# Low parts, token loads and the fifth group's norm in another order in a channel mixer on one core

## The chip, the cores and the metric

The kernel runs on one core of a Trainium2 chip. The metric is device time in microseconds (us) of the whole program. The engines are PE (TensorE, matrix products), DVE (VectorE), ACT (ScalarE), POOL (GpSimd) and SP (SyncE, which here only issues DMA transfers).

## The reference

Three stages follow each other. The first is a linear attention with softmaxes over q and k; its output is x. The second and third are the ones that the change touches:

```python
def _moe_ref(x, w_tok1, w_tok2, w_ch1, w_ch2):
    h = np.maximum(x.transpose(0, 2, 1) @ w_tok1, 0.0) @ w_tok2
    u = x + h.transpose(0, 2, 1)
    h2 = np.maximum(u @ w_ch1, 0.0) @ w_ch2          # 512 -> 1536 -> 512   ("stage B")
    return u + h2

def _moe2_ref(x, g_ln, w_ch1, w_ch2):
    mu = np.mean(x, axis=-1, keepdims=True)
    var = np.mean((x - mu) ** 2, axis=-1, keepdims=True)
    xn = (x - mu) / np.sqrt(var + 1e-06) * g_ln
    ch = np.maximum(xn @ w_ch1, 0.0) @ w_ch2         # 512 -> 2048 -> 512   ("stage C")
    return x + ch
```

There are 8 x 576 = 4608 tokens of 512 channels, all in fp32.

## The kernel before

**Phase A** (up to about 224 us of the span) does the attention and the token mixing. **The plain stage** (224 to 350 us) does stage B for the first of five token groups with ordinary products, in 12 units of weights, while the weights of stages B and C are prepared for the rest.

**The calls** (350 us to the end) do the other nine positions: position 1 to 4 is stage B for token groups 1 to 4, position 5 to 9 is stage C for all five groups. A group is 2 x 462 tokens (2 x 456 for the last). A large product of 2 x 2 blocks is done with seven block products instead of eight (Winograd's form), so that each call has seven products p = 0 to 6. A position has a few *mixing-in calls* j = 0, 1, ... (three in B, four in C; the product with w1) and then one *w2 call* (j < 0; the product with w2). Each product of a mixing-in call is one *entry*; each product of a w2 call is three entries in B and four in C. One entry is one weight tile of 512 KB in a ring of four (`w_ring`) and twelve matmuls. Entries of a call are counted from 0 (n).

Every operand stands as a high part and a low part (`x_hi` and `x_lo`, `o_hi` and `o_lo`): three matmuls (lines 1445 to 1447) make one exact product of them. ACT writes the high part, and DVE then the low one as the difference. The operands of x are seven (p = 0 to 6); four sums (`sum_x`) on DVE stand between them. Each of the nine positions prepares the x of the next one: p = 0 to 3 in the last mixing-in call, the rest behind it. The operands of the hidden layer are made entry by entry (`hi_o` on ACT, `lo_o` on DVE, line 1308), with `sum_o` (lines 1294 to 1302) before products 2, 4 and 6. `take` (ACT line 886, DVE line 1278) brings a product from PSUM to the hidden layer, `relu` (line 892) and `relu_t1` (line 1285) finish it, and `take_y` (line 1320) adds the products of a w2 call to the result. PE may start product p when product p - 2 has been taken.

All order is written out by hand. Each engine runs through the calls in the same order of steps, and executes its own instructions strictly one after another; semaphores tie them. SP issues, at each entry, first the weight tile four entries on (when PE is done with this entry), then what else falls there: `load_x` (line 428; the four quarters of the x of two positions on, into the single tile `xn`), `load_res` (line 473), and stores of y. All of these go through SP's one DMA queue. POOL adds the weight blocks and stores and loads the weight units (lines 590, 557, 558) through its own queue.

**The norm** of stage C is spread over the mixing-in calls of the position before, by the table `NORM_AT`: (j, p) is the call and product at which each step stands. Its mean and variance are sums over channels made by PE (`moment 0`, `moment 1`, four small matmuls each). The first row of the table is for the norm of position 5, which is made during position 4 (here "the fifth's norm"); the other row is for the later ones. `HI_AT` is the list of entries at which ACT makes the high parts of a weight unit; its last number is that of the last unit, in position 4.

Of the kernel before, what the change touches and what calls it, by code (L numbers as in the profile page):

```python
# [8 lines left out]
def mixer_kernel(nc, q, k, kT, v, w_tok1, w_tok2, w1b, w2b, g_ln, w1c, w2c, out):  # L9
# [45 lines left out]
    for pos in range(1, NX):  # L55
        stage, sg = "BC"[pos // NSG], pos % NSG
        for j in range(G1S[stage] + 1):
# [19 lines left out]
         "deviation 0": (0, 4), "deviation 1": (0, 4), "deviation 2": (0, 5), "deviation 3": (0, 5),  # L77
         "square 0": (0, 5), "square 1": (0, 5), "square 2": (0, 5), "square 3": (0, 5),
         "squares 01": (0, 6), "squares 23": (0, 6), "squares": (0, 6), "second high": (0, 6), "second low": (1, 0),
         "moment 1": (1, 2), "variance": (1, 3), "root": (1, 3), "newton": (1, 4),  # L80
         "scaled 0": (1, 5), "scaled 1": (1, 5), "scaled 2": (1, 6), "scaled 3": (1, 6)},
# [6 lines left out]
    HI_AT = ((0, 8, 27), (1, 6, 11, 27), (1, 6, 11, 27), (4,))  # L88
# [72 lines left out]
    with ctx:  # L161
# [201 lines left out]
        def _(sp):  # L363
# [159 lines left out]
            for c in CALLS:  # L523
                for n in range(7 * c.epp):
# [9 lines left out]
                    if c.j == 0 and c.pos == 1 and p in (2, 3, 4, 5):  # L534
                        load_x(2, p - 2)
                    if c.j < 0 and c.pos + 2 < NX and c.pos != NSG - 1 and p in (2, 3, 4, 5) and e == 0:
                        load_x(c.pos + 2, p - 2)
# [139 lines left out]
        def _(act):  # L677
# [70 lines left out]
            def plain(n):  # L748
# [25 lines left out]
                for p in {7: (0, 1), 8: (2, 3), 9: (4, 5), 10: (6,)}.get(n, ()):  # L774
                    hi_x(1, p)
# [156 lines left out]
            for c in CALLS:  # L932
# [21 lines left out]
                else:  # L954
                    for n in range(7 * c.epp):
# [4 lines left out]
                        if c.pos + 1 < NX and n in (c.epp, c.epp + 2):  # L960
                            hi_x(c.pos + 1, 5 + (n > c.epp))
# [3 lines left out]
        def _(dve):  # L965
# [165 lines left out]
            def plain(n):  # L1131
# [17 lines left out]
                if n == 6:  # L1149
                    sum_x(1, 0)  # L1150
                    lo_side(2)
                if n == 7:
                    lo_x(1, 0)
                    lo_x(1, 1)
                    sum_x(1, 1)
                if n == 8:
# [3 lines left out]
                if n == 9:  # L1160
# [3 lines left out]
                if n == 10:  # L1164
# [220 lines left out]
            for c in CALLS:  # L1385
                after = CALLS[c.index + 1] if c.index + 1 < len(CALLS) else None
                split = c.pos + 1 < NX
                if c.j >= 0:
                    last = c.j == G1S[c.stage] - 1
                    for p in range(7):  # L1390
                        if p == 0 and c.j > 0:
                            relu_t1(CALLS[c.index - 1])
                        if p in (3, 4, 5):
# [12 lines left out]
                        if last and split and p == 4:  # L1406
                            lo_x(c.pos + 1, 2)
                            lo_x(c.pos + 1, 3)
                        if last and p == 5:
                            lo_o(after, 0, 0)  # L1410
                            lo_o(after, 0, 1)
                        if last and split and p == 6:
                            lo_x(c.pos + 1, 4)
                        if last and p == 6 and after.epp > 3:
                            lo_o(after, 0, 2)
                else:
                    for n in range(7 * c.epp):
# [12 lines left out]
                        if split and n == c.epp:  # L1430
                            lo_x(c.pos + 1, 5)
# [285 lines left out]
```

## Time and profile before

| | us |
|---|---|
| median of 3 runs | 1524.27 (1522.53 to 1527.17) |
| the profiled execution, its own time | 1519.46 |
| span of the profiled execution (first to last instruction) | 1517.7 |
| PE busy | 1475.5 (97%) |
| DVE busy | 1048.5 (69%) |
| ACT busy | 687.0 (45%) |
| POOL busy | 266.9 (18%) |

The profiled execution is 4.8 us below the median of the runs. A PE matmul is shown with a modelled duration that overlaps the next one, so its pace is read from start to start and not from the duration.

### The profile page before, as it was taken

The page shows a single profiled execution, that of the slowest core. Times are in us where ns is not written, and L with a number is a line of the kernel's source. Part 1 is how long each engine was busy: PE and PEld are TensorE (multiplying, and loading weights), DVE is VectorE, ACT ScalarE, POOL GpSimd, SP SyncE. Part 2 cuts the span into 40 slices and gives each one's busy share as a digit, 9 for nine tenths or more (in the row PEclk, how much of TensorE's full clock was granted, in tenths as well). Part 3 has the DMA queues.
Part 4 walks back from the last instruction along what each step waited for, and adds up shares of the span by engine and source line. Part 5 has one row for each costly group of instructions (what it writes and reads, how often), then busy time and mean ns, then how long its engine had stood idle before and what let it go on. Part 6 is the DMA issues. An engine that isn't in the chain of part 4 may idle for free.

```text
span 1517.7 us, 19961 instructions
## 1 busy us (share of the span) xinstructions
PE 1475.5 (97%) x7656; PEld 1331.4 (88%) x7656; DVE 1048.5 (69%) x1187; ACT 687.0 (45%) x862; POOL 266.9 (18%) x280
## 2 busy tenths in 40 slices
PE   6999999998999999999999999999999999999998
PEld 6999998887888888888888888888888888889997
DVE  7989874593693782785975786588568756872276
ACT  5656564452543633634533443454245324532342
POOL 5454656652121222110000000000000000000000
PEclk9999999999999999999999999999999999999999
DMA  7788849889889999987777768766866787678766
GB/s 240 244 265 243 277 167 332 334 319 368 310 326 313 371 328 312 342 320 256 251 261 265 239 227 271 238 233 236 277 238 219 257 257 254 203 232 249 250 210 201
DMA packets 138719, 407.27 MB, mean 268 GB/s; under 512 B 13568, under 2 KB 35392, under 8 KB 138624
## 3 DMA queue, kind: packets, MB, share of 16 engines
q1 hardware_dynamic: 123024, 347.00, 68.1%
q0 software_dynamic: 15600, 58.99, 10.5%
q8 instruction: 62, 1.02, 0.3%
q14 instruction: 33, 0.27, 0.1%
HBM read 326.24 MB, written 79.69 MB: 267 GB/s over the span
## 4 chain that ended last, share of the span: by engine, by line
PE 81%; DMA 8%; DVE 6%; issue 2%; POOL 1%; ACT 1%; SPq 0%; DVEq 0%; ACTq 0%; POOLq 0%
PE ps L1445 26%; PE ps L1447 26%; PE ps L1446 25%; DMA w_ring<-w_scratch_B 4%; DMA w_scratch_B<-w_out 3%; PE ps L1469 1%; DVE x_lo L1066 1%; PE ps L1560 1%; PE ps L1480 1%; DVE o_lo L1308 1%; DMA vt<-v 0%; DVE k_max L971 0%; DVE w_out L1113 0%; DVE kv L1027 0%; DVE h L1278 0%
## 5 line engine op out<-in xcount | busy, mean ns | idle before, releaser
L1445 PE MATMUL ps<-x_hi,w_ring 128*128 128x462 f32 (+1 forms) x920 | 343.9, 374 | 12.6 <-DMA w_ring<-w_scratch_B 7.8
L1445 PE MATMUL ps<-o_hi,w_ring 128*128 128x462 f32 (+1 forms) x920 | 343.1, 373 | 5.8 <-DVE o_lo L1308 3.2
L1447 PE MATMUL ps<-x_hi,w_ring 128*128 128x462 f32 (+1 forms) x920 | 342.8, 373 | 0.0
L1446 PE MATMUL ps<-o_lo,w_ring 128*128 128x462 f32 (+1 forms) x920 | 341.6, 371 | 0.0
L1447 PE MATMUL ps<-o_hi,w_ring 128*128 128x462 f32 (+1 forms) x920 | 341.5, 371 | 0.0
L1446 PE MATMUL ps<-x_lo,w_ring 128*128 128x462 f32 (+1 forms) x896 | 333.5, 372 | 0.0
L907 ACT CAST o_hi<-h 128x924 fp32r<-128x924 f32 (+1 forms) x189 | 182.0, 963 | 235.3 <-PE ps L1447 223.5
L1308 DVE TENSOR_TENSOR o_lo<-h,o_hi 128x924 fp32r<-128x924 f32 (+1 forms) x189 | 212.4, 1125 | 63.2 <-ACT o_hi L907 63.1
L1445 PEld LDWEIGHTS ps<-x_hi,w_ring 128*128 128x128 f32 x920 | 173.5, 189 | 38.2 <-issue 13.0
L1445 PEld LDWEIGHTS ps<-o_hi,w_ring 128*128 128x128 f32 x920 | 173.1, 188 | 32.8 <-issue 12.3
L1447 PEld LDWEIGHTS ps<-x_hi,w_ring 128*128 128x128 f32 x920 | 173.4, 188 | 19.5
L1446 PEld LDWEIGHTS ps<-o_lo,w_ring 128*128 128x128 f32 x920 | 173.2, 188 | 19.2
L1447 PEld LDWEIGHTS ps<-o_hi,w_ring 128*128 128x128 f32 x920 | 173.0, 188 | 19.2
L1278 DVE TENSOR_TENSOR h<-ps,h 128x924 f32<-128x924 f32 (+1 forms) x81 | 90.5, 1117 | 139.0 <-PE ps L1447 138.8
L1446 PEld LDWEIGHTS ps<-x_lo,w_ring 128*128 128x128 f32 x896 | 169.5, 189 | 19.0
L886 ACT ACTIVATE h<-ps 128x924 f32<-128x924 f32 (+1 forms) x108 | 101.4, 940 | 179.6 <-PE ps L1447 179.5
L892 ACT ACTIVATE h<-h 128x924 f32<-128x924 f32 (+1 forms) x54 | 52.7, 975 | 161.7 <-DVE h L1278 161.7
L1320 DVE TENSOR_TENSOR res<-ps,res 128x924 f32<-128x924 f32 (+1 forms) x63 | 70.1, 1113 | 55.0 <-PE ps L1447 54.3
L1066 DVE TENSOR_TENSOR x_lo<-xn,x_hi 128x924 fp32r<-128x924 f32 (+1 forms) x63 | 70.9, 1139 | 22.0 <-ACT x_hi L798 22.0
L798 ACT CAST x_hi<-xn 128x924 fp32r<-128x924 f32 (+1 forms) x63 | 59.3, 957 | 11.0 <-DVE xn L1050 7.1
L590 POOL DMA_DIRECT2D w_scratch_C<-w_out x13 | 12.5, 960 | 282.2 <-DVE w_out L1171 282.2
L907 ACT CAST o_hi<-last_pair 128x924 fp32r<-128x924 f32 (+1 forms) x35 | 33.8, 965 | 45.3 <-PE ps L1447 45.3
(172 smaller groups left out, 2132.7 us busy)
## 6 DMA issues: line engine op xcount, KB each, us to landing
w_ring<-w_scratch_C SPq DMA_DIRECT2D x280, 512.0 KB, 3.8
w_ring<-w_scratch_B SPq DMA_DIRECT2D x168, 512.0 KB, 5.0
w_scratch_C<-w_out POOLq DMA_DIRECT2D x13, 1792.0 KB, 11.4
w_scratch_B<-w_out POOLq DMA_DIRECT2D x12, 1792.0 KB, 10.6
kt<-kT SPq DMA_DIRECT2D x32, 288.0 KB, 6.1
u_scratch<-u_out SPq DMA_DIRECT2D x32, 288.0 KB, 3.3
qt<-q SPq DMA_DIRECT2D x32, 256.0 KB, 4.8
ke<-k SPq DMA_DIRECT2D x32, 256.0 KB, 5.0
```

The source lines that it names most:

```text
L798: nc.scalar.copy(x_hi[:, p, :, 0:n], x).then_inc(x_hi_made, 1)
L886: nc.scalar.activation(hidden(dst, c.j, c.n), bank[:, :, 0:c.n], func)\
L892: nc.scalar.activation(x, x, ACT.Relu).then_inc(relu_made, 1)
L907: nc.scalar.copy(o_hi[:, g % RO, :, 0:c.n], hidden((0, 1, 1, 2, 0, 3, 3)[p], e, c.n)).then_inc(o_hi_made, 1)
L1066: nc.vector.tensor_tensor(x_lo[:, p, :, 0:n], x, x_hi[:, p, :, 0:n], ALU.subtract)\
L1278: nc.vector.tensor_tensor(x, bank[:, :, 0:c.n], x, ALU.add).then_inc(taken["dve"], 1)
L1308: nc.vector.tensor_tensor(o_lo[:, g % RO, :, 0:c.n], src, o_hi[:, g % RO, :, 0:c.n], ALU.subtract)\
L1320: nc.vector.tensor_tensor(y, bank[:, :, 0:c.n], y, ALU.add).then_inc(taken["dve"], 1)
L1445: mm(dst, a_hi, b_hi, start=start, stop=False, skip_group_check=onto)
L1446: mm(dst, a_hi, b_lo, start=False, stop=False, skip_group_check=onto)
L1447: return mm(dst, a_lo, b_hi, start=False, stop=stop, skip_group_check=onto)
L1469: x = mm(dst, ke[:, t, c * P:(c + 1) * P], vt[:, t, c // 2, c % 2 * P:c % 2 * P + P + 1], start=t == 0, stop=t == NT - 1)
```

## The change

It changes no computation, only when things are done, in five places.

1. DVE, last mixing-in call of each position: the low part of the w2 call's first operand (`lo_o(after, 0, 0)`) stands before the take of product 5 and not behind it; `lo_x` 3, 4, 5, `sum_x` 3 and `lo_x` 6 each move back, to product 6 and to entries epp, epp + 1, epp + 2 and epp + 4 of the w2 call (epp is 3 in B and 4 in C). ACT makes the high part 6 one entry later.
2. SP, w2 calls: the four quarters of the x of two positions on are loaded at products 3, 4, 5, 6 and not at 2, 3, 4, 5.
3. SP, position 1: the four quarters for position 2 are loaded at entries 4, 6, 8, 10 and not at 2, 3, 4, 5.
4. The fifth's norm: deviations and squares one product earlier, "second high" behind the take of product 0 of call j = 1, variance, root, newton and the scalings one product earlier; the last weight unit's high part at entry 0 and not 4.
5. Plain stage: x operands one unit later.

```diff
-         "deviation 0": (0, 4), "deviation 1": (0, 4), "deviation 2": (0, 5), "deviation 3": (0, 5),
-         "square 0": (0, 5), "square 1": (0, 5), "square 2": (0, 5), "square 3": (0, 5),
-         "squares 01": (0, 6), "squares 23": (0, 6), "squares": (0, 6), "second high": (0, 6), "second low": (1, 0),
-         "moment 1": (1, 2), "variance": (1, 3), "root": (1, 3), "newton": (1, 4),
-         "scaled 0": (1, 5), "scaled 1": (1, 5), "scaled 2": (1, 6), "scaled 3": (1, 6)},
+         "deviation 0": (0, 3), "deviation 1": (0, 3), "deviation 2": (0, 4), "deviation 3": (0, 4),
+         "square 0": (0, 3), "square 1": (0, 3), "square 2": (0, 4), "square 3": (0, 4),
+         "squares 01": (0, 5), "squares 23": (0, 5), "squares": (0, 6), "second high": (1, 0), "second low": (1, 0),
+         "moment 1": (1, 2), "variance": (1, 2), "root": (1, 2), "newton": (1, 3),
+         "scaled 0": (1, 4), "scaled 1": (1, 4), "scaled 2": (1, 5), "scaled 3": (1, 5)},
...
-    HI_AT = ((0, 8, 27), (1, 6, 11, 27), (1, 6, 11, 27), (4,))
+    HI_AT = ((0, 8, 27), (1, 6, 11, 27), (1, 6, 11, 27), (0,))
...
-                    if c.j == 0 and c.pos == 1 and p in (2, 3, 4, 5):
-                        load_x(2, p - 2)
-                    if c.j < 0 and c.pos + 2 < NX and c.pos != NSG - 1 and p in (2, 3, 4, 5) and e == 0:
-                        load_x(c.pos + 2, p - 2)
+                    if c.pos == 1 and (c.j, p) in ((0, 4), (0, 6), (1, 1), (1, 3)):
+                        load_x(2, ((0, 4), (0, 6), (1, 1), (1, 3)).index((c.j, p)))
+                    if c.j < 0 and c.pos + 2 < NX and c.pos != NSG - 1 and p in (3, 4, 5, 6) and e == 0:
+                        load_x(c.pos + 2, p - 3)
...
+                        if last and p == 5:
+                            lo_o(after, 0, 0)
+                        if last and p == 6 and after.epp > 3:
+                            lo_o(after, 0, 2)
                         if p in (3, 4, 5):
                             take(c, p)
...
                         if last and split and p == 4:
                             lo_x(c.pos + 1, 2)
-                            lo_x(c.pos + 1, 3)
                         if last and p == 5:
-                            lo_o(after, 0, 0)
                             lo_o(after, 0, 1)
                         if last and split and p == 6:
-                            lo_x(c.pos + 1, 4)
-                        if last and p == 6 and after.epp > 3:
-                            lo_o(after, 0, 2)
+                            lo_x(c.pos + 1, 3)
...
                         if split and n == c.epp:
+                            lo_x(c.pos + 1, 4)
+                        if split and n == c.epp + 1:
                             lo_x(c.pos + 1, 5)
-                        if split and n == c.epp + 1:
+                        if split and n == c.epp + 2:
                             sum_x(c.pos + 1, 3)
-                        if split and n == c.epp + 2:
+                        if split and n == c.epp + 4:
                             lo_x(c.pos + 1, 6)
```

The first place is SP's list at the start of the calls, position 1. `w_ring` is a weight tile, `y_scratch<-res` a store of the plain stage's result, `xn` a quarter of the x of position 2. Before:

```order
L463 DMA w_ring<-w_scratch_B 128x1024
L485 DMA y_scratch<-res 128x924 x4
L463 DMA w_ring<-w_scratch_B 128x1024 x3
L428 DMA xn<-u_scratch 128x924
L463 DMA w_ring<-w_scratch_B 128x1024
L428 DMA xn<-u_scratch 128x924
L463 DMA w_ring<-w_scratch_B 128x1024
```

In the change:

```order
L463 DMA w_ring<-w_scratch_B 128x1024 x5
L428 DMA xn<-u_scratch 128x924
L463 DMA w_ring<-w_scratch_B 128x1024 x2
L428 DMA xn<-u_scratch 128x924
L463 DMA w_ring<-w_scratch_B 128x1024 x2
```

The tiles of entries 7 and 8 had one and two quarters of x ahead of them that are now behind them.

The second place is DVE's list at the end of a last mixing-in call in stage C (takes of products 4 and 5 are the `last_pair` rows of L1278). Before:

```order
L1278 TENSOR_TENSOR last_pair<-ps,last_pair 128x924
L1066 TENSOR_TENSOR x_lo<-xn,x_hi 128x924 x2
L1278 TENSOR_TENSOR last_pair<-ps,last_pair 128x924
L1308 TENSOR_TENSOR o_lo<-h,o_hi 128x924 x2
L1066 TENSOR_TENSOR x_lo<-xn,x_hi 128x924
```

In the change (its lines stand one or two further down):

```order
L1279 TENSOR_TENSOR last_pair<-ps,last_pair 128x924
L1066 TENSOR_TENSOR x_lo<-xn,x_hi 128x924
L1309 TENSOR_TENSOR o_lo<-h,o_hi 128x924
L1279 TENSOR_TENSOR last_pair<-ps,last_pair 128x924
L1309 TENSOR_TENSOR o_lo<-h,o_hi 128x924 x2
L1066 TENSOR_TENSOR x_lo<-xn,x_hi 128x924
```

The first `o_lo` of the w2 call has changed places with the fourth `x_lo`; the take of product 5 still has two instructions ahead of it, and the second `o_lo` still follows that take.

The third place is ACT's list in the fifth's norm, from the takes of products 0 and 1 of call j = 0 in position 4 on. L782 is the last weight unit's high part, L892 a relu, L919 the squares, L923 "second high". Before:

```order
L886 ACTIVATE h<-ps 128x2x456 x2
L916 CAST s_hi<-ln 128x924
L886 ACTIVATE h<-ps 128x2x456
L892 ACTIVATE h<-h 128x2x456
L782 CAST w_out<-w_op 128x7x256
L892 ACTIVATE h<-h 128x2x456
L919 ACTIVATE ln<-xn 128x924 x4
L886 ACTIVATE h<-ps 128x2x456
L923 CAST s_hi<-ln 128x924
L886 ACTIVATE h<-ps 128x2x456 x3
```

In the change:

```order
L782 CAST w_out<-w_op 128x7x256
L886 ACTIVATE h<-ps 128x2x456
L916 CAST s_hi<-ln 128x924
L886 ACTIVATE h<-ps 128x2x456
L919 ACTIVATE ln<-xn 128x924 x2
L892 ACTIVATE h<-h 128x2x456
L919 ACTIVATE ln<-xn 128x924 x2
L892 ACTIVATE h<-h 128x2x456
L886 ACTIVATE h<-ps 128x2x456 x2
L923 CAST s_hi<-ln 128x924
L886 ACTIVATE h<-ps 128x2x456 x2
```

The take of product 0 of call j = 1 (the second of the last "x2" before "second high") now stands ahead of "second high", and the squares are split in two pairs.

## Rows read from the trace of the kernel before

**Rows 1.** The page: busy time by engine; the chain that ended last.

```profile
PE 1475.5 (97%) x7656; PEld 1331.4 (88%) x7656; DVE 1048.5 (69%) x1187; ACT 687.0 (45%) x862; POOL 266.9 (18%) x280
...
PE 81%; DMA 8%; DVE 6%; issue 2%; POOL 1%; ACT 1%; SPq 0%; DVEq 0%; ACTq 0%; POOLq 0%
```

**Rows 2.** Windows: length, busy (count) by engine, granted clock, DMA share, GB/s.

```profile
362.00:370.00 8.00, 6.83 (x33) 5.80 (x32) 3.36 (x3) 2.89 (x3) 0.70 (x1) 1.00 1.03 420
713.79:718.00 4.21, 4.21 (x13) 3.72 (x14) 0.27 (x1) 0.77 (x1) 0.00 (x0) 0.59 0.86 311
900.00:1000.00 100.00, 100.00 (x478) 89.48 (x477) 65.08 (x61) 37.48 (x40) 0.00 (x0) 1.00 0.78 258
```

**Rows 3.** SP and PE timeline, position 1: start, length, engine, instruction.

```profile
357.92 0.42 SPq L428 DMA_DIRECT2D xn<-u_scratch  x1
360.05 0.32 SPq L463 DMA_DIRECT2D w_ring<-w_scratch_B  x1
360.42 0.81 SPq L428 DMA_DIRECT2D xn<-u_scratch  x1
...
369.88 0.45 PE L1445 MATMUL ps<-x_hi,w_ring 128*128 128x462 f32 x1 [1.17 <-DMA w_ring<-w_scratch_B]
...
372.27 0.37 PE L1447 MATMUL ps<-x_hi,w_ring 128*128 128x462 f32 x1
374.40 0.44 PE L1445 MATMUL ps<-x_hi,w_ring 128*128 128x462 f32 x1 [1.76 <-DMA w_ring<-w_scratch_B]
```

**Rows 4.** The chain in order of time around 370 us.

```profile
363.73 10.54 DMA w_ring<-w_scratch_B
```

**Rows 5.** Timeline around the start of the w2 call of position 5.

```profile
868.60 2.14 DVE L1066 TENSOR_TENSOR x_lo<-xn,x_hi 128x924 fp32r<-128x924 f32 x2
870.66 1.11 DVE L1278 TENSOR_TENSOR last_pair<-ps,last_pair 128x924 f32<-128x924 f32 x1
871.69 1.11 DVE L1308 TENSOR_TENSOR o_lo<-h,o_hi 128x924 fp32r<-128x924 f32 x1
872.21 0.38 PE L1447 MATMUL ps<-x_hi,w_ring 128*128 128x462 f32 x1
872.95 0.45 PE L1445 MATMUL ps<-o_hi,w_ring 128*128 128x462 f32 x1 [0.36 <-DVE o_lo L1308]
...
873.66 1.12 DVE L1308 TENSOR_TENSOR o_lo<-h,o_hi 128x924 fp32r<-128x924 f32 x1 [0.87 <-ACT o_hi L907]
```

**Rows 6.** Windows of DVE: second low part to that of entry 6, w2 calls, B.

```profile
409.56:424.08 14.52, 14.52 (x15) 1.00 0.79 272
519.49:534.66 15.17, 14.61 (x15) 1.00 0.82 284
```

**Rows 7.** DVE and PE timeline around entry 8, w2 call of position 1.

```profile
428.23 1.11 DVE L1308 TENSOR_TENSOR o_lo<-h,o_hi 128x924 fp32r<-128x924 f32 x1
...
429.49 0.45 PE L1445 MATMUL ps<-o_hi,w_ring 128*128 128x462 f32 x1
```

**Rows 8.** Windows of PE, entries 6 to 14 of the w2 calls of positions 1 and 3.

```profile
424.23:448.53 24.30, 23.39 (x109) 1.00 0.93 338
...
647.84:671.82 23.98, 23.20 (x108) 1.00 0.91 327
```

**Rows 9.** Timeline of DVE, ACT and PE in the fifth's norm.

```profile
710.79 1.12 DVE L1366 TENSOR_TENSOR ln<-ln 128x924 f32<-128x924 f32 x1
...
711.94 0.96 ACT L923 CAST s_hi<-ln 128x924 fp32r<-128x924 f32 x1 [2.03 <-DVE ln L1366]
712.81 1.75 ACT L886 ACTIVATE h<-ps 128x912 f32<-128x912 f32 x2
...
710.03 0.37 PE L1447 MATMUL ps<-x_hi,w_ring 128*128 128x456 f32 x1
713.79 0.47 PE L1445 MATMUL ps<-x_hi,w_ring 128*128 128x456 f32 x1 [3.39 <-ACT h L886]
```

**Rows 10.** DVE timeline, the first of the three steps of "newton", and the take before.

```profile
723.95 1.11 DVE L1278 TENSOR_TENSOR h<-ps,h 128x912 f32<-128x912 f32 x1 [0.35 <-PE ps L1447]
724.97 1.11 DVE L1375 TENSOR_TENSOR ln<-ln 128x924 f32<-128x924 f32 x1
```

More of the change, by code:

```diff
@@ L773, in plain @@
                     hi_side(2)
-                for p in {7: (0, 1), 8: (2, 3), 9: (4, 5), 10: (6,)}.get(n, ()):
+                for p in {8: (0, 1), 9: (2, 3), 10: (4, 5), 11: (6,)}.get(n, ()):
                     hi_x(1, p)
@@ L959, in _ @@
                             hi_unit(HI_AT[c.e0 + n])
-                        if c.pos + 1 < NX and n in (c.epp, c.epp + 2):
+                        if c.pos + 1 < NX and n in (c.epp, c.epp + 3):
                             hi_x(c.pos + 1, 5 + (n > c.epp))
@@ L1149, in plain @@
                 if n == 6:
-                    sum_x(1, 0)
                     lo_side(2)
                 if n == 7:
+                    sum_x(1, 0)
+                if n == 8:
                     lo_x(1, 0)
@@ L1155, in plain @@
                     sum_x(1, 1)
-                if n == 8:
+                if n == 9:
                     lo_x(1, 2)
@@ L1159, in plain @@
                     lo_x(1, 3)
-                if n == 9:
+                if n == 10:
                     lo_x(1, 4)
@@ L1163, in plain @@
                     sum_x(1, 3)
-                if n == 10:
+                if n == 11:
                     lo_x(1, 6)
```

## The prediction

> **What bounds the kernel now.** I read the page first: PE is busy for 97% of the span and holds 81% of the chain that ended last; DMA holds 8% and DVE 6% [rows 1]. So only what makes PE wait counts. The windows give PE's undisturbed pace: 478 matmuls in 100 us, 0.21 us each, 2.52 us for an entry of twelve [rows 2]. I then went through PE's starts and looked at each step longer than 0.21 us. Those steps are few, and the change touches four sets of them.
>
> (a) In position 1 entries 7 and 8 start at 369.88 and 374.40, each on a landed weight tile [rows 3]. The second start comes 2.13 us after the matmul before it and so is 1.92 late; the first is 1.34 late: its row shows 1.17 of idleness behind a modelled end that lies 0.16 (0.37 - 0.21) after the free start, as 1.76 + 0.16 gives the 1.92 of the second. The tile of entry 8 took 10.54 us to land [rows 4].
>
> (b) At the start of the w2 calls of positions 1 to 8 (eight times) PE's step is about 0.74 us, 872.21 to 872.95, and the row names the low part o_lo as releaser [rows 5]. That is 0.53 late. A first matmul after a wait also has a step of about 0.28 and not 0.21, so a wait costs 0.6 in all.
>
> (c) In the w2 calls of positions 1 to 3 the nine entries from entry 6 on take 24.30 us (position 1) and 23.98 (position 3), against 9 x 2.52 = 22.7 [rows 8]; position 2 is like them. Most of the 1.3 to 1.6 us excess is weight tiles that land late, at entry 12 above all, with DMA at 91% and 93% of its time.
>
> (d) In the fifth's norm PE steps from 710.03 to 713.79, 3.55 us late, and waits for a take on ACT [rows 9]. That take stood behind "second high", which waited 2.03 us for the sum of squares on DVE. Right behind the wait the granted clock is 0.59 on average over 4.21 us, in which 13 matmuls fit where 20 would (4.21 / 0.21) [rows 2]; part of that stretch is at 1.2 GHz, half the full 2.4.
>
> **The change, part by part.**
>
> *Weight tiles of position 1.* A quarter of x is 128 x 924 x 4 bytes, 0.47 MB; at the 420 GB/s of 362 to 370 us it takes 1.1 us, and about twice that while POOL's queue carries a weight store too [rows 2]. The quarters issued at 357.92 and 360.42 stand in SP's queue ahead of the tiles of entries 7 (issued 360.05) and 8 [rows 3]. With both behind, tile 7 comes up to 2.2 us sooner, more than the 1.34 that it is late, and tile 8 some 4 us sooner, more than the 1.34 + 1.92. The quarters now fall at entries 4, 6, 8 and 10, one every 5 us, and x is wanted only at entry 14, three entries (7.6 us) after the last. Gain 3.3 and 2 x 0.08 of slow first matmuls: **3.5**. If the tiles are late for POOL's store and not for x, it is 0; the whole is 3.5.
>
> *Start of the w2 calls.* DVE runs two x_lo (868.60, 2.14 us), the take (870.66), then o_lo (871.69), whose end at 872.80 releases PE 0.15 us later [rows 5]. In the change o_lo stands after the first x_lo and ends at about 870.7, 1.7 us before PE's free start at 872.42. The take stays where it was, behind two instructions. What is late next is the second low part: it waits for ACT (relu of product 5, then the high part), as before at 873.66, ends at 874.78 and lets PE go at 874.93, where PE wants 872.42 + 2.52 = 874.94 [rows 5]. It just fits. In C DVE then has gaps, and the wait vanishes in four calls: 4 x 0.6 = **2.3**. Bounds 0 and 2.4.
>
> In B it does not pay. From the second low part to that of entry 6 DVE works 14.52 of 14.52 us in position 1 [rows 6]; positions 3 and 4 are the same within 0.13. The change puts the same number of instructions into this stretch, which begins when the second high part is there, at the old time. So PE starts the w2 call 0.5 sooner and waits it off by entry 6. Only position 2 has a gap there, 15.17 - 14.61 = 0.56 [rows 6], a take_y that waited for a load; SP issues that load after entry 1, now 0.5 sooner: **0.5**.
>
> *The seventh x_lo in B.* It leaves entry 5 (sum_x 3 takes the place) for entry 7, where it stands behind a weight unit's low part and ahead of take_y and the low part of entry 8. That one ends at 429.34 now and PE starts on it at 429.49 [rows 7], already 0.15 late. One DVE instruction more, 1.03 from start to start as between 870.66 and 871.69 [rows 5], makes PE 1.03 later in positions 1, 2 and 3. If nothing else changed this would cost **3.1**.
>
> *x loads a product later.* In the same calls the first quarter stood ahead of the tile of entry 12, the late one. Behind it, that tile lands at least 1.1 sooner, and PE comes 1.03 later to it. The excess of the nine entries (1.6, 1.4 and 1.3) should shrink to the DVE wait alone, 0.15 + 1.03 + 0.08 = 1.26: gains of 0.4, 0.15 and 0.05, **0.6** after the 3.1 is paid. Later, at entry 18, the queue carries only tiles and one store; x is next wanted in the following position (stage C: at its call 0, three entries on; the fifth's norm: two entries and a take_y on, some 6 us).
>
> *The fifth's norm.* The take of product 0 now precedes "second high", so PE's 3.55 wait goes, and with it the slow stretch: 4.21 - 13 x 0.21 = 1.5 [rows 2, 9]. The squares come one product earlier too. New: the three steps of newton now stand between the takes of products 3 and 4. By my count PE runs product 2 at 710.2, its moment ends at 713.7, variance 715.0, root 716.0, take 3 at 716.2 to 717.3, newton 717.2 to 720.65 (three at 1.15, like the one at 724.97 [rows 10]), take 4 ends 721.7, and PE wants it at 721.0: 0.9 late. Bounds 0 and 2.5 (all three steps plus the take, none hidden). Gain 5.05 - 0.95: **4.1**. The Trainium skill (TensorE: Matmul & The Clock Gate, section "Part 1: The HAM clock gate") says that the number of slow matmuls at the start of activity differs from run to run; by that the 1.5 need not be paid in every run, and the sum would be 9.5 in the runs that escape it. One trace can't tell.
>
> *Plain stage.* The x operands move by one unit of 10 us; the last low part ends some 3 us before PE's first call. Nothing: the cover is that unit's products. Without cover it would be 1 us.
>
> Sum: 3.5 + 2.3 + 0.5 + 0.6 + 4.1 = **11.0**. The profiled execution's 1519.46 becomes 1508.5; the median of the runs stands 4.8 above its profile, and the same 11.0 off it is **1513.3**. What this kernel's measurement can tell from no change is about 0.3%, 4.6 us.
>
> **The rivals.**
>
> *The queue keeps its debt.* DMA is at 91 to 103% in all these stretches [rows 2, 8]; tiles may be late because of the total. Then (a) gives nothing and the three entry-8 waits are paid in full on top of the late tiles: 11.0 - 3.5 - 3.7 = 3.8, time 1520.5, no telling from before. Against it: where PE runs without a wait DMA needs 78% of its time [rows 2], so what is moved out of a crowded stretch finds room in the next. Chance 0.10.
>
> *DVE hands the wait on.* The second low part has a margin of 0.01; if it comes 0.3 to 0.6 late in C, (b) is worth 0 to 1. With newton at its worst, 2.5, the sum is 11.0 - 2 - 1.5 = 7.5, time 1516.8. For it: DVE without a gap in B [rows 6]. Chance 0.18.
>
> *SP stands still: slower.* The first quarter of x waits on SP for the seventh x_lo, and the weight tiles queue behind it. Now x_lo 6 is at entry 7 and the quarter at entry 9, six calls of this kind. If x_lo 6 ended after the tiles' reserve (entry 9, plus three tiles in the ring), each us would be PE's. By rows 7 it ends near 428.3 and SP gets there near 434.8, so 6.5 us are spare, and the ring's reserve on top. It decides only from 2.6 us of PE time per call (6 x 2.6 = 15.6, over 11.0 + 4.6): time 1529. Chance 0.03.
>
> *It doesn't act.* Each of PE's waits has another cause just behind, and all but the norm's 4.1 stays: 1520.2. Chance 0.05.
>
> **How the numbers follow.** The forecast has 0.64. Its own range is 1510.5 to 1515.5 (the bounds of newton and of C). The range of 1509.5 to 1520 takes in the DVE rival and most of the queue's. Faster by over 0.3% means below 1519.7: 0.64 + 0.18 and a little of the others, 0.84; slower 0.04; same 0.12.
>
> **What would show it.** PE's step at 369.88 and 374.40 back to 0.21; the eight w2 calls of B and C starting without a wait, entry 6 in B as late as before; a new wait of about 1.2 at entry 8 in positions 1 to 3 and none at entry 12; no clock below 1.00 near 714; a wait of some 0.9 before product 6 of call j = 1 of position 4. I am wrong if entries 7 to 9 of position 1 still wait for DMA, or if PE's time at entry 12 in B is later than before.

## The result and the profile after

The changed kernel takes 1517.4 us (median of 11 runs, 1509.66 to 1519.65) against 1524.3 for the kernel before in the same comparison (11 runs, 1521.35 to 1533.88). The ratio is 0.995, 95% interval 0.9936 to 0.9964: faster by 7.6 us of 1524.27, with the interval from 5.5 to 9.8. The forecast was 11.0 us and 1513.3.

The profiled execution of the changed kernel took 1519.06, which is 1.7 above its median, while that of the kernel before was 4.8 below its own. So the two traces differ by 1.2 us of span (1517.7 and 1516.5) where the medians differ by 6.9. The traces can show single waits. They can't show the total.

The page of the changed kernel: span; busy time by engine; the chain; and the two groups of matmuls that begin an entry, where the last columns are idle time ahead of them and what ended it. For these two groups the rows of the kernel before stand ahead. Lines of the changed kernel stand one or three further down: 1448 to 1450 are the three matmuls, 1309 is `lo_o`, 1279 the take on DVE, 1321 `take_y`.

```profile
span 1516.5 us, 19961 instructions
...
PE 1473.3 (97%) x7656; PEld 1330.2 (88%) x7656; DVE 1047.1 (69%) x1187; ACT 686.8 (45%) x862; POOL 265.3 (17%) x280
...
PE 69%; DMA 5%; DVE 4%; issue 1%; ACT 0%; SPq 0%; DVEq 0%
...
L1445 PE MATMUL ps<-x_hi,w_ring 128*128 128x462 f32 (+1 forms) x920 | 343.9, 374 | 12.6 <-DMA w_ring<-w_scratch_B 7.8 <-ACT h L886 3.4 <-issue 1.4
L1445 PE MATMUL ps<-o_hi,w_ring 128*128 128x462 f32 (+1 forms) x920 | 343.1, 373 | 5.8 <-DVE o_lo L1308 3.2 <-issue 1.8 <-DMA w_ring<-w_scratch_B 0.5
...
L1448 PE MATMUL ps<-x_hi,w_ring 128*128 128x462 f32 (+1 forms) x920 | 343.6, 373 | 9.5 <-DMA w_ring<-w_scratch_B 7.9 <-issue 1.0 <-DVE h L1279 0.6
L1448 PE MATMUL ps<-o_hi,w_ring 128*128 128x462 f32 (+1 forms) x920 | 343.2, 373 | 8.6 <-DVE o_lo L1309 6.6 <-issue 1.0 <-DMA w_ring<-w_scratch_B 1.0
```

PE does the same matmuls as in [rows 1]. ACT's 3.4 us, the take of the fifth's norm, is gone. The waits for weight tiles are not less in total: 7.9 and 1.0 us, where the kernel before has 7.8 and 0.5. Those for low parts have grown from 3.2 to 6.6 us: the waits at the starts of the w2 calls are gone and others, inside the w2 calls of stage B, have come, as the next views show.

From PE start to PE start, the two traces compare so (us, before and after; "6 to 9" are the entries n of a w2 call):

| stretch | pos. 1 | pos. 2 | pos. 3 | pos. 4 |
|---|---|---|---|---|
| mixing-in calls | 59.13, 56.06 | 55.12, 55.81 | 58.48, 58.55 | 59.80, 55.75 |
| w2 call, entries 0 to 6 | 15.39, 15.92 | 16.04, 16.98 | 15.37, 17.00 | 15.26, 15.80 |
| 6 to 9 | 7.86, 8.89 | 7.85, 8.91 | 7.85, 8.90 | 7.55, 7.66 |
| 9 to 15 | 16.44, 16.52 | 16.21, 15.50 | 16.14, 15.35 | 14.91, 14.91 |
| 15 to the next position | 15.12, 15.12 | 15.12, 15.12 | 15.12, 15.12 | 15.55, 17.03 |

The first row runs to the start of the w2 call and so holds the wait there, 0.50 to 0.55 in the kernel before. The mixing-in calls of positions 5 to 8 are shorter by 0.59, 0.57, 0.51 and 0.50. Phase A is 1.06 longer and the plain stage 0.61 shorter. Over the fourteen traces these two vary by 3.5 and 3.2 us, though every edit lies behind phase A. The plain stage has one of the five edits; no kernel here makes that one alone. It takes 119.9 us on average in the five traces without the edit and 119.0 in the nine with it, single traces 117.5 to 120.7, so a gain of 1 us there is neither shown nor excluded. A single difference below about 1 us in this table is no evidence by itself; one that repeats in three or four places is.

Timeline of the changed kernel around the start of the w2 call of position 5, to hold against [rows 5]:

```profile
869.55 1.11 DVE L1066 TENSOR_TENSOR x_lo<-xn,x_hi 128x924 fp32r<-128x924 f32 x1
870.58 1.12 DVE L1309 TENSOR_TENSOR o_lo<-h,o_hi 128x924 fp32r<-128x924 f32 x1
871.61 1.12 DVE L1279 TENSOR_TENSOR last_pair<-ps,last_pair 128x924 f32<-128x924 f32 x1
...
872.73 0.38 PE L1448 MATMUL ps<-x_hi,w_ring 128*128 128x462 f32 x1
873.37 0.37 PE L1448 MATMUL ps<-o_hi,w_ring 128*128 128x462 f32 x1
```

The two PE rows are three matmuls apart, 0.64 = 3 x 0.21: the w2 call starts without a wait, its low part having ended 1.7 earlier, at 871.70. This is so in all eight.

Timeline of the changed kernel around entry 8 in position 1, to hold against [rows 7]:

```profile
423.96 1.21 DVE L1172 TENSOR_TENSOR w_out<-w_op,w_out 128x1024 fp32r<-128x1024 f32 x1
425.10 1.11 DVE L1066 TENSOR_TENSOR x_lo<-xn,x_hi 128x924 fp32r<-128x924 f32 x1
426.13 1.11 DVE L1321 TENSOR_TENSOR res<-ps,res 128x924 f32<-128x924 f32 x1
427.16 1.10 DVE L1309 TENSOR_TENSOR o_lo<-h,o_hi 128x924 fp32r<-128x924 f32 x1
...
428.41 0.45 PE L1448 MATMUL ps<-o_hi,w_ring 128*128 128x462 f32 x1 [1.02 <-DVE o_lo L1309]
```

DVE has no gap; the second row is the seventh x_lo. PE starts 1.17 late here (a step of 1.38 from start to start, less 0.21), 1.18 and 1.15 in positions 2 and 3.

SP, PE and the chain of the changed kernel, start of position 1, to hold against [rows 3, 4] (in the last row: start and duration of the transfer):

```profile
357.99 5.81 SPq L463 DMA_DIRECT2D w_ring<-w_scratch_B  x3
363.85 0.60 SPq L428 DMA_DIRECT2D xn<-u_scratch  x1
366.00 2.86 SPq L463 DMA_DIRECT2D w_ring<-w_scratch_B  x2
368.91 0.44 SPq L428 DMA_DIRECT2D xn<-u_scratch  x1
...
374.88 0.45 PE L1448 MATMUL ps<-x_hi,w_ring 128*128 128x462 f32 x1 [1.38 <-DMA w_ring<-w_scratch_B]
...
366.00 8.75 DMA w_ring<-w_scratch_B
```

Entries 7 and 8 start freely. The tile of entry 9 has one quarter of x ahead of it (three in the kernel before), took 8.75 us, and makes PE 1.54 late, since PE now comes to it sooner.

The fifth's norm in the changed kernel, to hold against [rows 9, 10]: timeline rows of DVE, ACT and PE.

```profile
709.67 1.12 DVE L1367 TENSOR_TENSOR ln<-ln 128x924 f32<-128x924 f32 x1
...
711.76 0.93 ACT L886 ACTIVATE h<-ps 128x912 f32<-128x912 f32 x1 [2.36 <-PE ps L1450]
712.59 0.95 ACT L923 CAST s_hi<-ln 128x924 fp32r<-128x924 f32 x1
...
708.99 0.44 PE L1448 MATMUL ps<-x_hi,w_ring 128*128 128x456 f32 x1 [0.63 <-DMA w_ring<-w_scratch_B]
...
723.39 1.12 DVE L1380 SCALAR_TENSOR_TENSOR ln<-ln 128x924 f32<-128x924 f32 x1
724.43 1.10 DVE L1279 TENSOR_TENSOR h<-ps,h 128x912 f32<-128x912 f32 x1
...
725.59 0.48 PE L1448 MATMUL ps<-x_hi,w_ring 128*128 128x456 f32 x1 [0.58 <-DVE h L1279]
```

ACT now takes first and waits only for PE, so the wait of 3.55 is gone. Two small ones are there instead: 0.78 for a weight tile at product 0 (708.99) and 0.74 for the take behind newton (725.59). Windows of the changed kernel (columns as in [rows 2]):

```profile
611.74:615.80 4.06, 4.06 (x12) 3.53 (x13) 3.46 (x4) 0.35 (x1) 0.96 (x1) 0.58 0.93 364
...
708.00:718.00 10.00, 9.37 (x46) 8.21 (x45) 5.33 (x6) 5.36 (x7) 0.00 (x0) 1.00 0.76 266
```

The clock stays at 1.00 through the norm. A stretch at 0.58 has appeared at 611.74, behind a wait of 1.98 for a weight tile that the trace of before does not have.

### The profile page after: what moved, and what is told of

Read it like the earlier page. It is cut to its first block, busy times and chain, and to the rows that moved or that the text cites. A ratio compares the mean times of both kernels' runs of the same rounds, so it can differ in the third digit from the quotient of the medians.

```text
span 1516.5 us, 19961 instructions
## 1 busy us (share of the span) xinstructions
PE 1473.3 (97%) x7656; PEld 1330.2 (88%) x7656; DVE 1047.1 (69%) x1187; ACT 686.8 (45%) x862; POOL 265.3 (17%) x280
## 4 chain that ended last, share of the span: by engine, by line
PE 69%; DMA 5%; DVE 4%; issue 1%; ACT 0%; SPq 0%; DVEq 0%
PE ps L1448 23%; PE ps L1450 23%; PE ps L1449 23%; DMA w_ring<-w_scratch_B 5%; DVE o_lo L1309 2%; DMA res<-u_scratch 1%; DVE x_lo L1066 1%; DVE h L1295 1%; DVE res L1321 0%; DVE h L1279 0%; PE ps L1597 0%; PE ps L1598 0%; DVE w_out L1172 0%; DVE h L1286 0%; ACT h L892 0%
## 5 line engine op out<-in xcount | busy, mean ns | idle before, releaser
L892 ACT ACTIVATE h<-h 128x924 f32<-128x924 f32 (+1 forms) x54 | 52.7, 975 | 158.1 <-DVE h L1279 158.0
```

The lines of the kernel that those rows point to most:

```text
L892: nc.scalar.activation(x, x, ACT.Relu).then_inc(relu_made, 1)
```

## The experiments

My theory of the gain was the four terms of the prediction. The rivals were that only some of them act, and that weight tiles in crowded stretches keep their lateness whatever is moved. The first four kernels do one part of the change each, on the kernel before; the plain stage's edit has no such kernel.

**DVE order alone** (edit 1 of the change, nothing else).

> The kernel before with the new DVE order alone (first o_lo ahead of the take, x_lo 3 to 6 and sum_x 3 moved back). Theory (each of PE's waits has its own cause and adds up): the eight waits at the start of a w2 call vanish; in stage C this gives 4 x 0.6 = 2.3 us and stays; in stage B it is waited off by entry 6, and entry 8 of positions 1 to 3 waits 1.2 us (3 x 1.03 more), part of which the late weight tiles behind it cover. Sum between 2.3 faster and 0.8 slower, about 1 us faster. Rival (DVE hands the wait on): the second product of the w2 calls in C waits 0.3 to 0.6 us instead, and the whole is 1 to 3 us slower.

Measured: 1523.11 (12 runs), ratio 1.0002 [0.9983, 1.0021]. In the trace the C calls start 0.56, 0.57, 0.54 and 0.50 sooner, and entry 8 is late by 1.18 and 1.16 in positions 2 and 3. In position 1 it is only 0.19 late: PE had waited 2.0 at entry 5 and then ran at a clock of 0.66 for 5 us, while DVE went on. So entry 8 costs 2.2 in this trace and 3.1 where it is late three times. Against the 2.2 won in C that leaves no gain, as measured.

**Position 1's x loads alone** (edit 3).

> The kernel before with the x loads of position 1 alone moved to entries 4, 6, 8 and 10. Theory: entries 7 and 8 start without a wait, 3.5 us faster, visible in the mixing-in calls of position 1 and nowhere else. Rival (the queue keeps its debt): the same tiles or the next ones are late by as much, total within 1 us of before. The changed kernel's trace already shows entry 9 waiting 1.54 us, so I expect 2 to 3 us rather than 3.5.

Measured: 1521.29 (12 runs), 0.9974 [0.9959, 0.9988]: faster by 4.0, interval 1.8 to 6.2. The trace gives 2.2 of it in position 1 (59.13 to 56.91): the tiles of entries 7 and 8 land 7.2 and 7.3 us after their issue, not 9.7 and 10.5. It also shows where the rest of the forecast 3.5 stayed, in one PE row of its timeline, entry 9:

```profile
375.88 0.45 PE L1445 MATMUL ps<-x_hi,w_ring 128*128 128x462 f32 x1 [1.48 <-DMA w_ring<-w_scratch_B]
```

**x loads of the w2 calls alone** (edit 2).

> The kernel before with the x loads of the w2 calls alone at products 3 to 6. Theory: the late tile at entry 12 of positions 1 and 3 comes in time, 1.3 + 1.1 + 1.1 us less at most over positions 1 to 3; about 2 us faster. Rival (the queue keeps its debt): tiles are late elsewhere, no change. Second rival: the later x loads meet the weight store of the next position's first unit and cost there, 0 to 2 us slower.

Measured: 1522.16 (12 runs), 0.9985 [0.9969, 1.0001]: no gain shown. The first quarter of x now stands behind the tile of entry 12, which lands in 7.6 us in position 1, not 8.3. But in this trace the tile of entry 14 is then the late one (PE timeline, position 1):

```profile
447.70 0.47 PE L1445 MATMUL ps<-o_hi,w_ring 128*128 128x462 f32 x1 [1.11 <-DMA w_ring<-w_scratch_B]
```

Position 1 waits 0.38 and 1.26 at the two, position 2 0.31 and 1.19. Over three positions in each of the traces, entries 9 to 15 take 16.26 us on average with the old loads (four kernels), and 16.22 and 16.57 with the new ones (four kernels, and this one). So the lateness as a whole did not shrink. That the order moved it from one tile to the next is not shown: in position 1 the tile of entry 12 takes 8.1 us on average in the four traces with the old loads and 8.2 in the ten with the new, and entry 14 is late in some traces with the old loads too (1.09 in the kernel with the norm alone).

**The fifth's norm alone** (edit 4).

> The kernel before with the fifth's norm (and the last weight unit) alone moved. Theory: the 3.55 us wait and the slow clock behind it go, a wait of 0.75 before product 6 of call j = 1 comes, 4 us faster in the mixing-in calls of position 4. Rival (the last weight unit's store, now 14 us earlier, makes weight tiles late): a further wait of about 0.8 us at product 0 of call j = 1, as the changed kernel's trace has it, 3.3 us faster.

Measured: 1521.07 (12 runs), 0.9977 [0.9961, 0.9993]: faster by 3.5, interval 1.1 to 5.9. Position 4's mixing-in calls go from 59.80 to 56.60. Waits of 1.07 at product 0 and 0.73 behind newton, as in the changed kernel. The other three kernels of this group keep the old norm. In each the wait of 3.55 stands there again with a slow clock behind it; windows of the kernels with the DVE order alone and with position 1's x loads alone:

```profile
724.85:729.06 4.21, 4.21 (x13) 3.70 (x14) 0.27 (x1) 0.77 (x1) 0.00 (x0) 0.59 0.86 296
...
716.08:720.29 4.21, 4.21 (x11) 3.73 (x12) 0.27 (x1) 0.77 (x1) 0.00 (x0) 0.50 0.87 310
```

The next four kernels take one suspected fault out of the changed kernel each.

**The seventh x_lo at entry 9 in stage B.**

```diff
-                        if split and n == c.epp + 4:
+                        if split and n == c.epp + (4 if c.epp > 3 else 6):
                             lo_x(c.pos + 1, 6)
```

> The changed kernel with x_lo 6 in stage B two entries later still (entry 9, where no weight unit's low part stands ahead of it; stage C as it is). Theory: the wait of 1.17 us before entry 8 of positions 1, 2 and 3 comes from this one DVE instruction and falls to 0.15; products 6 to 8 of these w2 calls take 7.86 and not 8.9 us. The late weight tiles at entries 12 and 14 may take up to 1 us each of it back: 1 to 3 us faster than the changed kernel, 0.6 to 0.7% under the kernel before. Rival (the wait is DVE's whole backlog): it moves to entry 9 or 10 and nothing is won.

Measured: 1510.97 (6 runs), 0.9925 [0.99, 0.995]. Its timeline at the place shown above:

```profile
426.21 1.11 DVE L1321 TENSOR_TENSOR res<-ps,res 128x924 f32<-128x924 f32 x1
427.24 1.11 DVE L1309 TENSOR_TENSOR o_lo<-h,o_hi 128x924 fp32r<-128x924 f32 x1
...
428.15 0.37 PE L1450 MATMUL ps<-o_hi,w_ring 128*128 128x462 f32 x1
428.50 0.45 PE L1448 MATMUL ps<-o_hi,w_ring 128*128 128x462 f32 x1
```

PE's step is 0.35: 0.14 late, as in [rows 7], and not 1.17. Entries 6 to 9 take 7.85 us in all three positions, 1.04, 1.06 and 1.05 less than in the changed kernel. Nothing behind it takes the 3.1 back: entries 9 to 15 average 16.20 in the traces without this wait and 16.22 in those with it. By the ratio the gain over before is 11.4 (7.6 to 15.2) against 7.6 (5.5 to 9.8). The two intervals overlap, so it is the trace that shows the 3.1, and the times agree with it.

**The `res` load out of entry 1.** In the changed kernel DVE's take_y at entry 5 of positions 2 and 3 waits for a quarter of `res` that SP loads after entry 1. Timeline of the changed kernel, position 2:

```profile
527.14 1.11 DVE L1295 TENSOR_TENSOR h<-h 128x924 f32<-128x924 f32 x1
530.05 1.12 DVE L1321 TENSOR_TENSOR res<-ps,res 128x924 f32<-128x924 f32 x1 [1.80 <-DMA res<-u_scratch]
...
532.35 0.45 PE L1448 MATMUL ps<-o_hi,w_ring 128*128 128x462 f32 x1 [1.12 <-DVE o_lo L1309]
```

```diff
-                    if c.stage == "B" and c.j == 2 and p in (2, 4, 6):
-                        load_res(c.pos, p // 2 - 1)
-                    if c.stage == "B" and c.j < 0 and n == 1:
-                        load_res(c.pos, 3)
+                    if c.stage == "B" and c.j == 2 and p in (0, 2, 4, 6):
+                        load_res(c.pos, p // 2)
```

> The changed kernel with the last quarter of the result tile in stage B loaded with the others, at products 0, 2, 4, 6 of the last mixing-in call and not at entry 1 of the w2 call. Theory: the waits of 1.3 us before entry 5 in positions 2 and 3 come from take_y waiting for this load, with the next low part queued behind it; they vanish, 2 to 2.5 us faster than the changed kernel. Rival (entry 5 waits for DVE's backlog): they stay. Second rival (queue debt): weight tiles in the mixing-in calls are late by as much, no gain.

Measured: 1514.94 (12 runs), 0.9947 [0.993, 0.9964], not to be told from the changed kernel. DVE's wait is gone (entries 0 to 6 take 15.34 and 15.29 in positions 2 and 3, not 16.98 and 17.00). Weight tiles of the mixing-in call before are late instead; two PE rows of its timeline, positions 2 and 3:

```profile
515.88 0.45 PE L1446 MATMUL ps<-x_hi,w_ring 128*128 128x462 f32 x1 [1.11 <-DMA w_ring<-w_scratch_B]
...
631.49 0.45 PE L1446 MATMUL ps<-x_hi,w_ring 128*128 128x462 f32 x1 [1.95 <-DMA w_ring<-w_scratch_B]
```

**Newton one product later.**

```diff
-         "newton": (1, 3), "scaled 0": (1, 4), "scaled 1": (1, 4), "scaled 2": (1, 5), "scaled 3": (1, 5)},
+         "newton": (1, 4), "scaled 0": (1, 5), "scaled 1": (1, 5), "scaled 2": (1, 6), "scaled 3": (1, 6)},
```

> The changed kernel with newton and the scalings of the fifth's norm back at the products they had. Theory: the wait of 0.74 before product 6 of call j = 1 in position 4 is the take of product 4 behind newton's three steps; it vanishes and nothing comes for it, 0.8 us faster in the mixing-in calls of position 4. Rival: the scalings, now later, make the x operands of position 5 late in call j = 2 and a wait of 0.5 to 1 comes there.

Measured: 1515.59 (9 runs), 0.995 [0.9933, 0.9967]. The take now precedes newton on DVE, and PE does not wait:

```profile
721.99 1.11 DVE L1279 TENSOR_TENSOR h<-ps,h 128x912 f32<-128x912 f32 x1 [1.38 <-PE ps L1450]
723.01 1.11 DVE L1376 TENSOR_TENSOR ln<-ln 128x924 f32<-128x924 f32 x1
```

Position 4's mixing-in calls take 54.68, 1.07 less: 0.74 of it is this wait, most of the rest the tile at product 0 (0.55 late, not 0.78). No new wait stands there. A gain of this size is under what the times can tell.

**The last weight unit's high part back at entry 4.**

```diff
-    HI_AT = ((0, 8, 27), (1, 6, 11, 27), (1, 6, 11, 27), (0,))
+    HI_AT = ((0, 8, 27), (1, 6, 11, 27), (1, 6, 11, 27), (4,))
```

> The changed kernel with the last weight unit's high part back at entry 4 of call j = 0 of position 4, the rest of the norm as changed. Theory (the wait of 0.8 to 1.1 at product 0 of call j = 1 is a weight tile slowed by this unit's store, 14 us earlier than before): that wait goes. But ACT and DVE then have the unit's work between the squares, so a wait of 1 to 2.5 us at products 1 or 2 of j = 1 comes back. Net 0.5 us faster to 2 us slower. Rival: the wait at product 0 stays, since it isn't this store.

Measured: 1515.68 (7 runs), 0.9943 [0.9922, 0.9964]. The wait at product 0 of call j = 1 is gone; PE passes the place in even steps:

```profile
707.33 0.37 PE L1450 MATMUL ps<-x_hi,w_ring 128*128 128x456 f32 x1
707.53 0.37 PE L1448 MATMUL ps<-x_hi,w_ring 128*128 128x456 f32 x1
```

Position 4's mixing-in calls take 54.87, 0.89 less. With the unit at entry 0 its store is under way just when this tile is loaded, here from 697.66 on; with the unit at entry 4 it follows. POOL timeline and windows, the changed kernel first:

```profile
697.66 0.95 POOL L590 DMA_DIRECT2D w_scratch_C<-w_out  x1 [32.60 <-DVE w_out L1172]
...
700.00:708.00 8.00, 8.00 (x41) 7.21 (x39) 7.76 (x8) 5.27 (x6) 0.00 (x0) 1.00 1.01 359
...
711.90 0.96 POOL L590 DMA_DIRECT2D w_scratch_C<-w_out  x1 [47.04 <-DVE w_out L1172]
...
700.00:708.00 8.00, 8.00 (x40) 7.22 (x40) 7.79 (x8) 5.46 (x6) 0.00 (x0) 1.00 0.71 226
```

The tile takes 8.79 us to land beside the store and 4.43 without it. All fourteen traces agree: 8.5 to 10.1 us and 0.49 to 2.05 late in the six with the unit at entry 0, 4.2 to 4.5 us and no wait in the eight with it at entry 4.

**Old DVE order in stage B, new order in C only.** This asks whether the first half of edit 1 is worth anything in B. Core of the edit, on the changed kernel:

```diff
-                        if last and p == 5:
+                        if last and p == 5 and c.stage == "C":
                             lo_o(after, 0, 0)
```

The x_lo 3 to 6, the sum_x and the second high part of x keep their old places in B too.

> The changed kernel with the new DVE order in stage C only; stage B has the order of before. Theory (in B the earlier start is waited off by entry 6, the new order buys nothing there and costs the entry-8 waits): PE waits 0.5 again at the start of the four w2 calls in B, entry 6 starts at the same distance from the last mixing-in call's product 6 as in the changed kernel, the entry-8 waits are 0.15; about 3 us faster than the changed kernel, less up to 1 us at the late tiles of entries 12 and 14, like the variant with x_lo 6 at entry 9. Rival (the new order helps in B too): 1 to 2 us slower than that variant.

Measured: 1514.24 (6 runs), 0.9933 [0.991, 0.9956]. The B calls start 0.52, 0.44, 0.39 and 0.55 late again, and entry 8 is 0.14 late as before. Against the kernel with x_lo 6 at entry 9 (0.9925) the times show no difference: as far as they reach, the new order buys nothing in B. This trace took 1522.43, 8.2 above its median, so only its single waits are read. The wait for `res` is there too, as in the kernels that move the x loads alone and have the old order throughout (entry 5 of position 2 is 2.3 and 1.8 late in them), and so does not come from the new order. DVE in position 1, and PE behind it:

```profile
419.70 1.12 DVE L1321 TENSOR_TENSOR res<-ps,res 128x924 f32<-128x924 f32 x1 [2.70 <-DMA res<-u_scratch]
...
422.00 0.45 PE L1460 MATMUL ps<-o_hi,w_ring 128*128 128x462 f32 x1 [2.26 <-DVE o_lo L1309]
```

**Three mends together** (x_lo 6 at entry 9 in B, newton later, unit at entry 4).

> The changed kernel with x_lo 6 at entry 9 in B, newton and the scalings at their old products, and the last weight unit at entry 4. Each was taken alone before. Theory (they act at different places and add up): no wait at entries 8 of positions 1 to 3, none at products 0 and 6 of call j = 1 in position 4: 3.1 + 0.8 + 0.8 less what late tiles take back, 3.5 to 4.7 us faster than the changed kernel, about 1512.5. Rival (unit and newton together fill DVE and ACT in j = 1): a wait of over 1 us comes at products 1 or 2 of j = 1, and it is no better than the variant with x_lo 6 alone.

Measured: 1509.76 (5 runs), 0.9905 [0.9892, 0.9919], 14.5 us faster than before. Its interval lies wholly below that of the changed kernel. In position 4 the two mends of the norm do not add up: the mixing-in calls take 54.69, no less than with newton alone (54.68), since the tile of product 5 of j = 1, loaded beside the store in its new place, is 0.58 late. The three together were expected to give 3.5 to 4.7 on top of the changed kernel; the times say 6.9, and with both intervals that is not apart from 4.7.

**The same with the `res` loads earlier.**

> The previous kernel with the last quarter of the result tile in B also loaded in the last mixing-in call. Theory: the waits before entry 5 (0.7 to 2.5 us in some w2 calls) vanish, and weight tiles of call j = 2 pay for it with as much: the same as without, within 1.5 us. Rival: a gain of 2 us.

Measured: 1511.41 (6 runs), 0.9912 [0.9896, 0.9928]: no gain on top, again. The tiles at the two places just shown for the `res` edit are 1.38 and 2.52 late here.

**The three mends, and position 1's x loads one entry later.**

```diff
-                    if c.pos == 1 and (c.j, p) in ((0, 4), (0, 6), (1, 1), (1, 3)):
-                        load_x(2, ((0, 4), (0, 6), (1, 1), (1, 3)).index((c.j, p)))
+                    if c.pos == 1 and (c.j, p) in ((0, 5), (1, 0), (1, 2), (1, 4)):
+                        load_x(2, ((0, 5), (1, 0), (1, 2), (1, 4)).index((c.j, p)))
```

> The combined kernel with the x loads of position 1 one entry later still: at entries 5, 7, 9 and 11. Theory (entry 9's tile is late because the first x quarter still stands ahead of it while POOL's queue carries its store and loads): the wait of 1.2 to 1.6 us before entry 9 of position 1 falls below 0.5, and about 1 us is won. Rival (the total of the transfers sets it): entry 9 or the next ones wait as long.

Measured: 1510.63 (5 runs), 0.9896 [0.988, 0.9911]. SP's and PE's rows at the place:

```profile
367.05 0.51 SPq L428 DMA_DIRECT2D xn<-u_scratch  x1
...
373.81 0.38 PE L1450 MATMUL ps<-x_hi,w_ring 128*128 128x462 f32 x1
374.02 0.37 PE L1448 MATMUL ps<-x_hi,w_ring 128*128 128x462 f32 x1
```

Entry 9 starts in step at 374.02, and entry 10 is only 0.13 late, against 1.54 at entry 9 in the changed kernel. But position 1's mixing-in calls take 55.86, only 0.74 less than without this edit, and 0.67 of that lies at entry 4, ahead of the moved loads: entry 16 is 1.06 late here (0.58 without). In the times it can't be told from the version without it.

## Why the prediction was right, and where it was not

Direction and the wide range were right. The size was 7.6 (5.5 to 9.8) where 11.0 was forecast, and 1517.4 lies outside the forecast's own range of 1510.5 to 1515.5. It lies nearest to the time of the rival "DVE hands the wait on" (1516.8), whose mechanism did not show; that the wide range holds it is in part luck. The terms as the changed kernel's trace has them are 2.5 (a), 2.2 (C) and 3.5 (norm), less 3.1 at entry 8: 5.1, a little under the measured interval. For (a) and the norm the 0.53 and 0.55 of the w2 call's start are taken off the first row of the table, since the w2 call gives them back by entry 6. Where the other 2.5 come from no trace shows; it is within what phase A, the plain stage and the late tiles vary by. Of the four parts timed alone, those of position 1 and of the norm carry the gain (4.0 and 3.5); the DVE order alone gives 0.

Both of the prediction's signs of being wrong came in part: entry 9 of position 1 waits for DMA, and PE reaches entry 12 in positions 2 and 3 later than before (551.97 and 667.13, not 550.53 and 664.18).

- **Start of the w2 calls.** Right: 2.17 in the four C calls for 2.3. In B the gain is waited off by entry 6 (+0.53 and +0.54 in positions 1 and 4), as predicted. Positions 2 and 3 lose more (0.94 and 1.63), by the late `res`.
- **Entry 8.** Right as a price: 1.03, 1.06 and 1.06 for 1.03 in each. Here one DVE instruction more on an engine without gaps was one PE wait of its length, and moving that one instruction removed it.
- **"x loads a product later."** This is the step that failed. The late tile at entry 12 was to come in time, repay the 3.1 and give 0.6 on top. Entries 9 to 15 take as long with either place of the loads (16.26, and 16.22 or 16.57), where 15.12 would be free of waits, so the 3.1 is paid in full: moving the loads gives about 0, where 3.1 + 0.6 = 3.7 was forecast. The "queue keeps its debt" rival was right here and, for the larger part, wrong for position 1. My argument was that 78% of DMA time is needed where PE runs freely, so that a next stretch has room. It did not hold inside a stretch at 91 to 93%. For this term I also counted only SP's queue: POOL's store of a weight unit is issued at 430.5 and takes 10.3 us in the kernel before, beside the tile of entry 12.
- **Tiles of position 1.** The mechanism was right and the size too large. Tiles 7 and 8 are in time; tile 9, which I had not priced, still has a quarter ahead of it and is 1.5 to 1.6 late. Alone the part gave 2.2 in the trace for 3.5. Putting the loads one entry later takes the wait at entry 9 away, but the calls of position 1 behind entry 4 are then only 0.1 shorter, since later tiles are late instead.
- **The norm.** Right but for one term: 3.5 in position 4 for 4.1, or 3.2 in the trace with this part alone. The 5.05 of wait and slow clock is gone, and newton costs 0.74 for 0.95. The tile beside the last unit's store, 0.8 and 1.1 in these two traces, was not foreseen: I had read that edit only as ACT's order and had not followed the store that it sets off.
- **Position 2's 0.5.** Missed. The load still lands late, in kernels of either order, and take_y waits 1.80 for it in the changed kernel.
- **The slow clock.** The 1.5 of the norm is a real term. A stretch at half clock stands behind the wait of 3.55 in all four traces that have this wait. Of the ten with the new norm one has such a stretch there, behind a tile 2.05 late. The mean granted clock of all runs says the same: 0.9965 for 35 runs of the kernel before and 0.9960 to 0.9970 for the three kernels that keep the old norm, but 0.9982 with the norm alone and 0.9989 in the changed kernel. In other places a slow stretch stands behind some waits of 2.0 to 2.5 and not behind others of the same length (2.53 in the kernel with the norm alone has one; 2.47 in that with newton later has none), and behind none of those of 1.5 at entry 9 and 1.3 at entry 5. The Trainium skill (TensorE: Matmul & The Clock Gate, "Part 1: The HAM clock gate") says that the number of slow matmuls at kernel start differs from run to run. At the 3.55 wait the traces do not bear that out: 13 matmuls in 4.21 us in three of them and 11 in the fourth, and no run that escapes it. At the shorter waits they do vary.
- **DVE hands the wait on, SP stands still, doesn't act.** None showed. The second low part of the C calls comes in time, and no call waits for SP behind x_lo 6.

Open: which transfer makes the tiles of entries 12 and 14 late. POOL's store of a weight unit runs beside them in its own queue. For the last unit such a store is shown to double a tile's landing time (4.4 to 8.8 us), but no kernel here moved the stores beside entries 12 and 14, so for these it is argued and not shown. The Trainium skill (DMA: Bandwidth & Descriptors, "Queues, rings and completion order") says that a DMA engine takes turns between the queues that have work for it. The 4.4 and 8.8 agree with that, but no run here shows the turns.

## What to carry to other kernels

Terms that rest on the order of instructions on one engine held to 0.3 us and repeated at each place. Count a wait for a transfer as gained only if the next transfers in the queue have slack. Here, in stretches with DMA above 90% busy, moving the x loads by a product won nothing, and moving the `res` loads made other tiles late; in position 1, where the loads were spread over twice the time, 2.2 of the forecast 3.5 was won. PE's waits for tiles added up to 8.3 us before and 8.9 after. For every moved instruction ask what stands behind it on its engine and which transfers it sets off; then mend the few places where the trace of the changed kernel shows a new wait, which here nearly doubled the gain (7.6 to 14.5 us). And when stretches of two traces are compared, see that a wait at their border is not counted as gained in one and lost in the next.

## What had not been expected of the hardware

Waits for transfers scatter between executions and kernels at places that no edit touches: the last entries of the w2 call of position 4 took 15.3 to 17.0 us, phase A 224.5 to 228.0, and the tile of product 6 of j = 1 in position 3 is up to 1.98 late (at 611.74 in the changed kernel) and in time in others. So one profiled execution stood 4.8 below its kernel's median and another 1.7 above it, more than most of the terms in the sum.

One store in another queue doubled the landing time of a single weight tile, 4.2 to 4.5 us without it and 8.5 to 10.1 beside it, in every one of fourteen traces. And behind PE's wait of 3.55 us the granted clock fell to half in four traces of four, so that this wait cost 5.05 us and not 3.55 in three of them, and more in the fourth.
